# An expert window of one token tile gets a program of its own: tokens stationary, weights moving

## The reference

```python
# 1. decayed linear attention, per batch and head (4 x 8, 768 steps, width 64)
state = gamma * state + outer(k[t], v[t]);  y[t] = scale * q[t] @ state
# 2. mixture of 8 experts, the best one for each token (D = 512, F = 1024)
e_idx = argmax(x @ w_gate + modality_bias[modality_id])
for e in range(8):
    h = relu(x[e_idx == e] @ w1[e])
    out[e_idx == e] = gate * (h @ w2[e])
# 3. a bilinear block
out = (((x @ w1) * (x @ w2)) @ w3) @ w_out
```

## Time and profile before

| | before |
|---|---|
| median of 3 runs | 889.22 us (887.43 to 889.95) |
| the profiled execution | 886.92 us, its span 885.2 us |
| PE busy | 858.8 us, 97% of the span |
| ACT busy | 239.4 us, 27% |
| DVE busy | 288.0 us, 33% |
| granted PE clock, mean | 0.991 |
| instructions | 14799 |

### The profile page before, as it was taken

One profiled execution on the slowest core, in us unless ns is written; L12 is line 12 of the kernel. 1 busy time (PEld: TensorE's weight loads), 2 busy tenths in 40 slices (PEclk: granted clock), 3 DMA queues, 4 the chain that ended last, 5 costly groups with the idle time before them and its releaser, 6 DMA issues.

```text
span 885.2 us, 14799 instructions
## 1 busy us (share of the span) xinstructions
PE 858.8 (97%) x5854; PEld 741.6 (84%) x5855; DVE 288.0 (33%) x499; ACT 239.4 (27%) x388; POOL 89.0 (10%) x111
## 2 busy tenths in 40 slices
PE   9999999998989999999989999999999999999995
PEld 8899888788989998888878888888888888888884
DVE  3678698411121422121425430230230230220210
ACT  2234423311212432112334421221221231221210
POOL 3232003120202020202000001001001001001001
PEclk9999999999999999999999999999999999999998
DMA  9999871531112052303146002002002002001000
GB/s 342 339 333 305 310 261 50 186 97 52 49 48 71 30 184 95 95 0 95 40 149 191 1 1 95 1 1 95 0 1 94 0 10 85 0 0 48 1 12 36
DMA packets 43094, 84.16 MB, mean 95 GB/s; under 512 B 7345, under 2 KB 7473, under 8 KB 43057
## 3 DMA queue, kind: packets, MB, share of 16 engines
q1 hardware_dynamic: 33376, 60.08, 19.6%
q0 software_dynamic: 4736, 14.72, 5.2%
q10 hardware_dynamic: 4946, 8.86, 3.0%
HBM read 62.64 MB, written 21.00 MB: 94 GB/s over the span
## 4 chain that ended last, share of the span: by engine, by line
PE 93%; DVE 3%; issue 2%; ACT 0%; ACTq 0%; POOL 0%; DVEq 0%
PE bank L398 47%; PE attn L398 33%; PE bank L793 3%; PE attn L820 3%; PE pair L805 3%; PE pair L898 1%; PE bank L832 1%; PE attn L811 1%; PE bank L770 1%; PE bank L950 1%; DVE w3T L1020 0%; DVE we_p L1020 0%; PE pair L777 0%; ACTq L353 0%; DVE hT L1266 0%
## 5 line engine op out<-in xcount | busy, mean ns | idle before, releaser
L398 PE MATMUL bank<-yT,wab 128*128 128x512 f32 x1152 | 262.2, 389 | 1.7 <-issue 1.7
L398 PEld LDWEIGHTS bank<-yT,wab 128*128 128x128 f32 x1152 | 216.1, 188 | 46.7 <-issue 1.9
L398 PE MATMUL bank<-xT,we_p 128*128 128x512 f32 (+2 forms) x768 | 154.2, 361 | 11.7 <-issue 8.0
L398 PEld LDWEIGHTS bank<-xT,we_p 128*128 128x128 f32 x768 | 136.8, 192 | 28.7 <-issue 10.4
L398 PE MATMUL attn<-hT,we_p 128*128 128x512 f32 (+2 forms) x768 | 153.5, 357 | 0.0
L398 PEld LDWEIGHTS attn<-hT,we_p 128*128 128x128 f32 x768 | 132.9, 188 | 14.4
L398 PE MATMUL attn<-wc,gT 128*128 128x512 f32 x576 | 131.5, 389 | 0.0
L398 PEld LDWEIGHTS attn<-wc,gT 128*128 128x128 f32 x576 | 108.1, 188 | 22.5
L1305 DVE TENSOR_TENSOR g<-bank,acopy 128x512 f32<-128x512 f32 x48 | 33.2, 692 | 258.8 <-PE bank L398 258.8
L1266 DVE SCALAR_TENSOR_TENSOR hT<-bank,hT 128x512 fp32r<-128x512 f32 x64 | 44.1, 691 | 171.5 <-ACT hT L659 171.5
L659 ACT ACTIVATE hT<-bank 128x512 fp32r<-128x512 f32 x64 | 38.2, 598 | 114.1 <-PE bank L398 114.1
(11 more groups left out here) (156 smaller groups left out, 572.0 us busy)
## 6 DMA issues: line engine op xcount, KB each, us to landing
we_raw<-in_moe_w_dram SPq DMA_DIRECT2D x6, 2048.0 KB, 9.1
yT_sorted<-yout ACTq DMA_DIRECT2D x8, 1024.0 KB, 4.9
qkv<-in_q_t_dram SPq DMA_DIRECT2D x24, 256.0 KB, 3.7
qkv<-in_v_dram SPq DMA_DIRECT2D x24, 256.0 KB, 5.4
x_rows<-x_keep SPq DMA_DIRECT2D x24, 256.0 KB, 3.3
ytile<-yT_sorted SPq DMA_DIRECT2D x6, 1024.0 KB, 5.0
qkv<-in_k_t_dram SPq DMA_DIRECT2D x23, 256.0 KB, 5.3
qkv<-in_k_dram SPq DMA_DIRECT2D x20, 256.0 KB, 5.8
```

The lines of the kernel that those rows point to most:

```text
L398: i = pe.matmul(out_, left(a), right(b), start=(first and n == 0), stop=(last and n == 2), **kw)
```

## The change

The `wide(2)` program goes. A window of two tiles uses `wide(3)` (there is none with these inputs), and a window of one tile gets a program of its own, `one_tile`, on PE, and matching branches on ACT and DVE:

- PE: h is made as tokens by features: for each half of 512 features 12 matmuls with the 128 tokens of `xT` stationary and w1 moving, 512 columns, into bank 0 or 1. ACT copies the bank to `h_rows`, PE transposes its four 128 x 128 blocks back into the same bank, ACT takes relu (one instruction for four blocks) and DVE the low part. Then 24 matmuls with `hT` stationary and w2 moving, 512 columns, make y as tokens by features in bank 4. ACT copies it to `y_rows`, PE transposes four blocks into bank 5, ACT copies that to `yout`, and the store writes 128 columns instead of 512.
- ACT and DVE read `SIZE` at the head of every window and branch on it. In the one-tile branch `w2_hi`/`w2_lo` for pieces 0 and 1 stand ahead of the h copies, and pieces 2 and 3 behind relu.
- In every window, the load of "the next window begins a new expert" (`coming`) is moved from f = 5 to behind f = 7, and the load of the first row (`start`) from the last y copy to ahead of the first.

```diff
+        def columns_of(tensor, start, wide=BANK):
@@ act
-                for f in range(KF):
-                    h_hi(w, f)
-                    if f == 0:
-                        this = is_new(act, w)
-                    if f in (1, 3):
-                        if_new(act, this, w, lambda run: w2_hi(run, range(f - 1, f + 1)))
-                    if f == KF - 3:
-                        coming = is_new(act, w + 1)
+                def wide_hidden():
...
+                def one_tile_hidden():
+                    this = is_new(act, w)
+                    if_new(act, this, w, lambda run: w2_hi(run, range(0, 2)))
+                    for half in range(2):
+                        act.wait_ge(s_hp, w * KF + (half + 1))
+                        copy(h_rows[:, half * BANK:(half + 1) * BANK], bank[half][:, :]).then_inc(s_hhi, 1)
+                    for half in range(2):
+                        act.wait_ge(s_hp, w * KF + (half + 1) * (GT - 1) + 2)
+                        act.activation(hT[:, HI, half * GT:(half + 1) * GT, 0:P], bank[half][:, :].rearrange("p (f t) -> p f t", f=GT),
+                                       ACT.Relu).then_inc(s_hhi, GT - 1)
+                    if_new(act, this, w, lambda run: w2_hi(run, range(2, 4)))
+                def one_tile_outward():
+                    act.wait_ge(s_yp, w * KD + 1)
+                    copy(y_rows[:, :], bank[4][:, :]).then_inc(s_y, 2)
+                    with act.If(total > w + 1):
+                        x_hi(w + 1, range(KD))
+                    act.wait_ge(s_yst, w * 16 + 16)
+                    act.wait_ge(s_yp, w * KD + KD)
+                    copy(yout[:, :, 0:P], bank[5][:, :].rearrange("p (d t) -> p d t", d=KD)).then_inc(s_y, 2)
+                    y_store(w, start, P)
+                    with act.If(total < w + 2):
+                        wab_hi(2)
+                        wab_hi(3)
+                size = table(act, w, SIZE, 1, GT)
+                with act.If(size > 1):
+                    wide_hidden()
+                with act.If(size < 2):
+                    one_tile_hidden()
+                coming = is_new(act, w + 1)
                 if_new(act, coming, w + 1, w1_hi)
                 with act.If(total < w + 2):
                     for j in range(KD):
                         yT_hi(0, j)
                     wab_hi(0)
                     wab_hi(1)
+                start = start_row(act, w)
+                with act.If(size > 1):
+                    wide_outward()
+                with act.If(size < 2):
+                    one_tile_outward()
@@ pe
+                def one_tile():
+                    run = table(pe, w, RUN_OF, 0, E - 1)
+                    for half in range(2):
+                        pe.wait_ge(s_hlo, w * KF + (half + 1))
+                        for k in range(KD):
...
+                            i = product(pe, bank[half][:, :], lambda a: xT[:, a, k, 0:P], lambda a: we1_p[:, a, k, half * BANK:(half + 1) * BANK],
+                                        k == 0, k == KD - 1)
+                        i.then_inc(s_hp, 1)
+                    for half in range(2):
+                        pe.wait_ge(s_hhi, w * KF + (half + 1))
+                        for t in range(GT):
+                            i = pe.transpose(bank[half][:, t * P:(t + 1) * P], h_rows[:, half * BANK + t * P:half * BANK + (t + 1) * P], ident)
+                        i.then_inc(s_hp, GT - 1)
+                    pe.wait_ge(s_y, w * KD + 1)
+                    for f in range(KF):
+                        if f % GT == 0:
+                            pe.wait_ge(s_hlo, w * KF + (f + GT + 2))
+                        if f % 2 == 0:
+                            pe.wait_ge(s_w2lo, run * (KF // 2) + (f // 2 + 1))
+                        i = product(pe, bank[4][:, :], lambda a: hT[:, a, f, 0:P], lambda a: we2_p[:, a, f, :], f == 0, f == KF - 1)
+                    i.then_inc(s_yp, 1)
+                    with pe.If(total > w + 1):
+                        x_rows(w + 1, range(KD))
+                    pe.wait_ge(s_y, w * KD + 4)
+                    for d in range(KD):
+                        i = pe.transpose(bank[5][:, d * P:(d + 1) * P], y_rows[:, d * P:(d + 1) * P], ident)
+                    i.then_inc(s_yp, KD - 1)
                 size = table(pe, w, SIZE, 1, GT)
...
-                    with pe.If(size > 2):
+                    with pe.If(size > 1):
                         wide(3)
-                    with pe.If(size < 3):
-                        wide(2)
+                    with pe.If(size < 2):
+                        one_tile()
@@ dve
+                def one_tile_hidden():
+                    this = is_new(dve, w)
+                    if_new(dve, this, w, lambda run: w2_lo(run, range(0, 2)))
+                    for half in range(2):
+                        dve.wait_ge(s_hhi, w * KF + (half + 1) * (GT - 1) + 2)
+                        fs = slice(half * GT, (half + 1) * GT)
+                        dve.scalar_tensor_tensor(hT[:, LO, fs, 0:P], bank[half][:, :].rearrange("p (f t) -> p f t", f=GT), 0.0,
+                                                 hT[:, HI, fs, 0:P].bitcast(F32), ALU.max, ALU.subtract).then_inc(s_hlo, GT)
+                    if_new(dve, this, w, lambda run: w2_lo(run, range(2, 4)))
+                size = table(dve, w, SIZE, 1, GT)
```

More of the change, by code:

```diff
@@ L206, in build @@
         hT = r("hT", [P, 2, KF, BANK], F32R)
+        h_rows = r("h_rows", [P, FF])
+        y_rows = r("y_rows", [P, DM])
         wab = region(at_w)("wab", [P, 2, 2, 2 * KD, BANK], F32R)
@@ L368, in start_row @@
             return 0 if isinstance(w, int) and w == 0 else table(eng, w, START, 0, NT * P)
-        def columns_of(tensor, start):
-            cols = tensor[:, start:start + BANK] if isinstance(start, int) else tensor[:, bass.ds(start, BANK)]
+        def columns_of(tensor, start, wide=BANK):
+            cols = tensor[:, start:start + wide] if isinstance(start, int) else tensor[:, bass.ds(start, wide)]
             return cols.rearrange("(d p) c -> p d c", p=P)
@@ L665, in y_copy, with y_store @@
                 copy(yout[:, d, :], bank[4 + d % 2][:, :]).then_inc(s_y, 1)
-            def y_store(w, start):
+            def y_store(w, start, wide):
                 act.wait_ge(s_y, w * KD + (KD + 2))
-                act.dma_start(columns_of(yT_sorted, start), yout[:, :, :]).then_inc(s_yst, 16)
+                act.dma_start(columns_of(yT_sorted, start, wide), yout[:, :, 0:wide]).then_inc(s_yst, 16)
             def wab_hi(f):
@@ L682, in window @@
             def window(w, total):
-                for f in range(KF):
-                    h_hi(w, f)
-                    if f == 0:
-                        this = is_new(act, w)
-                    if f in (1, 3):
-                        if_new(act, this, w, lambda run: w2_hi(run, range(f - 1, f + 1)))
-                    if f == KF - 3:
-                        coming = is_new(act, w + 1)
+                def wide_hidden():
+                    for f in range(KF):
+                        h_hi(w, f)
+                        if f == 0:
+                            this = is_new(act, w)
+                        if f in (1, 3):
+                            if_new(act, this, w, lambda run: w2_hi(run, range(f - 1, f + 1)))
@@ new lines, in wide_outward @@
+                def wide_outward():
+                    for d in range(KD):
+                        y_copy(w, d)
+                        if d < KD // 2:
+                            with act.If(total > w + 1):
+                                x_hi(w + 1, range(2 * d, 2 * d + 2))
+                        if d == 0:
+                            with act.If(total < w + 2):
+                                wab_hi(2)
+                                wab_hi(3)
+                    y_store(w, start, BANK)
@@ L932, in wide @@
                                 x_rows(w + 1, range(2 * d, 2 * d + 2))
+                def one_tile():
[3 more added lines that the diff above has]
+                        for k in range(KD):
+                            if half == 0:
+                                pe.wait_ge(s_ixlo, w * KD + (k + 1))
+                                pe.wait_ge(s_w1lo, run * KD + (k + 1))
+                            i = product(pe, bank[half][:, :], lambda a: xT[:, a, k, 0:P], lambda a: we1_p[:, a, k, half * BANK:(half + 1) * BANK],
[7 more added lines that the diff above has]
+                    pe.wait_ge(s_y, w * KD + 1)
+                    for f in range(KF):
+                        if f % GT == 0:
[7 more added lines that the diff above has]
+                    pe.wait_ge(s_y, w * KD + 4)
+                    for d in range(KD):
+                        i = pe.transpose(bank[5][:, d * P:(d + 1) * P], y_rows[:, d * P:(d + 1) * P], ident)
+                    i.then_inc(s_yp, KD - 1)
                 size = table(pe, w, SIZE, 1, GT)
@@ L1283, in window, with wide_hidden @@
             def window(w, total):
```

(16 more changed lines are left out.)

## The result

| | before | after |
|---|---|---|
| median | 889.37 us (887.43 to 889.95, 4 runs) | 880.38 us (876.75 to 881.25, 4 runs) |
| ratio to before | | 0.9895, 95% interval 0.9863 to 0.9926 |
| the profiled execution, its span | 886.92, 885.2 us | 881.25, 879.5 us |
| from window 0's first matmul to the end | 728.4 us | 720.7 us |
| granted PE clock, mean | 0.991 | 0.987 |

The forecast was 882.5, and the change takes 9 us off. The two profiles differ by only 5.7 us, because window 0 began 2.0 us later in the one of after (158.83 and not 156.83). That part of the program was not changed, and its start wandered between 156.2 and 159.9 us over the profiles of this study. I therefore count from window 0's first matmul on: 885.2 - 156.8 = 728.4 and 879.5 - 158.8 = 720.7, **7.7 us** less.

The account below looks back on a forecast made before the run. PE, busy 858.8 of 885.2 us, was taken as the bound. Stage 3 starting 8.3 us earlier, less 1.6 for one clock drop, gave 6.7 off 889.2: 882.5 us, overall range 874.5 to 886.5.

Parts of the forecast that it names:

- rival A: Code fetch ahead of window 2: dropping skipped wide(2) removes the 5.12 us gap and its clock drop, 6.7 us; chance 0.27.
- the likeliest case: Gaps ahead of windows 1 and 2 stand, one clock drop: 882.5 us, range 880 to 884.5; chance 0.52.
- The signs of being wrong: Gaps at windows 1 and 2 change, window 7 to stage 3 outside 18 to 22 us, or wide-window relu over 0.3 late.
- Steps 1 to 3: Window 7's h products, ACT's loads and copies, transposes, relu: PE waits 2.2 us for ACT; y products start at 465.45.
- Step 4: Window 7's y products: from 465.45 to 471.2, w2 pieces 2 and 3 just in time, margin under 0.3 us.
- the earlier pair of waits: PE's waits of 2.2 and 0.9 us in window 7, 461.1 to 465.45: second clock-drop candidate, left out of the sum.
- Step 5: End of window 7: ACT copies y behind stage-3 work and loads, so PE waits 1.9 us.
- Step 6: Loop end ahead of stage 3: 1.72 us of issue stays, at worst 5.12; stage 3 starts 8.3 us earlier.
- Step 7: Waits of 3.6 in 4.3 us right ahead of stage 3 bring one drop of PE's clock, costing 1.6 us.
- The wide windows: Seven windows of 384 or 512 columns: added and moved register loads cost 0, bound 2 us; dropping wide(2) costs nothing.
- Rival B: Window 7: second clock drop (1.6 us), exit 3.4 longer, or late w2 piece or load; 885.8 us; chance 0.15.
- Rival C: ACT's and DVE's longer loops fetch code in seven windows: 7 to 25 us, less 6.7; 896.5 us; chance 0.06.

Follow-up runs that it names:

- e5: Changed kernel with all four w2 pieces of the one-tile window moved behind relu and the low part, on ACT and DVE; 879.39 us, ratio 0.9910.
- e6: Changed kernel with ACT's and DVE's branch taken from the number of windows, without loading SIZE for it; 876.58 us, ratio 0.9883.
- e3: Changed kernel with matmuls of unused result put into PE's four waits of the one-tile window; 874.17 us, ratio 0.9863.
- e1: Changed kernel with the 256-column program put back in PE's loop body, where nothing runs it; 884.23 us, ratio 0.9976.
- e4: Changed kernel with all engines' window loops run exactly eight turns, without the five empty ones; 871.18 us, ratio 0.9808.
- e8: Kernel before with the window loops run exactly eight turns, without the five empty ones; 884.13 us, ratio 0.9964.
- e0: Kernel before, unchanged, run again for a second profile; 887.19 us.
- e2: Kernel before with only the 256-column program taken out, so the one-tile window runs the 384-column one; 886.72 us, ratio 0.9997.
- e10: Changed kernel, unchanged, run again for a second profile; 878.99 us, ratio 0.9891.
- e9: Changed kernel with exactly eight loop turns and filling matmuls in only PE's first three one-tile-window waits; 870.03 us, ratio 0.9803.
- e7: Changed kernel with both exactly eight loop turns and filling matmuls in PE's four one-tile-window waits; 870.62 us, ratio 0.9802.

## Why the prediction was right, point by point

The time, the sign and the range were right. The way there was right in part, and that the sum came within 2.1 us is luck, since two misses cancelled: the sum had 8.3 - 1.6 = 6.7 us from window 7 and the clock, which gave 5.4 - 2.9 = 2.5; rival A, which I had left out of the likeliest case, gave 6.3. The signs of being wrong that the prediction named did come. The gap at window 2 changed, and window 7 to stage 3 took 22.99 us, outside 18 to 22.

1. **Steps 1 to 3, the h half**: right. ACT's pieces began 3.8 us behind the store's issue (3.9 in the sum), PE waited 2.07 (2.2), and the y products began 9.9 us after the window's start (10.0). The remark that the order of ACT's branch costs most there was wrong: e5 turned it round and won nothing. The single price of a load, 1.0 us, was right for the first and too high for the next ones: taking one away gave 0.5 in e6.
2. **Step 4, the y products**: 8.36 us in place of 5.7. The term was missing because I left the earlier pair of waits out of the clock's account. In e3 and e1, where the clock stayed up, they took 5.78, so the products themselves and the just-in-time pieces of w2 were costed rightly.
3. **Step 5, the wait for the y copy**: 0.75 and not 1.9, and not only because the y products ended late: in e1 and e6, where they took 5.78 and 5.74, it was 0.75 too. ACT's loads of `coming` and `start` cost nothing, since its four `yT_hi` followed the w2 pieces at once (463.96, the pieces from 462.05, 2.00 long): those loads run beside its instructions. In the profile of after ACT even waited 2.51 us for PE.
4. **Step 6, the way out**: 3.35 and not 1.72, the failed step with the largest consequence. I had named both ends and taken the wrong one. The measured 1.72 was, by the simplest reading, what remained of the loop's end behind queued matmuls, and the new window ends with four short transposes. e4 and e8 show it from both sides: the same edit removes 3.35 in one kernel and 1.72 in the other.
5. **Step 7, the clock**: mechanism right, size wrong. Two spells and not one, and longer: 4 and 5 us had a mean of 0.69 and 0.66 in the earlier trace rows, and 5 and 6 us stayed at 0.50 in after. They cost 2.7 and 2.9 us, not 1.6 once. e3 removed both.
6. **The wide windows**: taken at 0, bound 2 us; the `SIZE` load showed 0.2 to 0.4 us in windows 2 and 3, gone in e6. `wide(2)`, "costs nothing when dropped", was the wrong sentence in the sum: its place in PE's loop body had cost 6.3 us, as rival A said.
7. **Rival A** (0.27) happened, by the mechanism given and at nearly the price given (6.7). **Rival B** (0.15), the second spell and the longer way out, happened too. I had treated them as cases that exclude each other, while they lie in different windows: the right list had a fourth entry, both at once, at the prices given 882.5 - 6.7 + 1.6 + 1.7 = 879.1, close to the 880.4 measured. **Rival C** (0.06) didn't happen: from window 3 to window 6 of after the longest "issue" wait of ACT is 1.0 us, ahead of the w1 pieces, where the load of `coming` now stands, and DVE has none. PE's longest wait there is 0.4 us.

The Trainium skill's rule behind C (Runtime: NRT & Kernel Launch, Instruction fetch mechanics), that a taken branch to code outside the pages held forces a fetch, agrees in kind with e0, e1 and e2: a program that is only skipped makes a gap of 4.3 to 5.1 us on PE, and the code queue moves more there. As to every turn it doesn't: between the windows from 3 to 7, with the same kind of turns and skips, no kernel here has an "issue" gap of even half a us.

## What to carry to other kernels

Before costing a branch that nobody takes at nothing, look at the "issue" gaps of the engine that is the bound: here the code that was skipped was worth more (6.3 us) than the code that was changed (2.5), and a loop run for its exact number of turns as much again in the changed kernel (3.35 and, through the clock, 3.1), though only 3.1 us in the kernel before. A gap measured behind a long row of queued matmuls is only what they left uncovered; where the new program ends in a few short instructions, take the whole. And when two rivals lie in different places, add a case in which both happen.

## What the runs showed of the hardware that I had not expected

- The empty turns of a loop on PE: 5 turns and the exit cost 3.4 us behind four transposes and 1.7 behind 96 matmuls of 256 columns, and nothing when they were left out.
- The lower clock comes in spells of differing length from the same waits: the y products took 8.38, 7.33, 8.21 and 8.15 us in after, e10, e4 and e5, and 5.78 and 5.74 in e1 and e6, with waits of about 2 and 1 us ahead of them in after, e10 and e1, 2.06 and 0.69 in e4, 1.54 and 1.07 in e6, 0.25 and 3.35 in e5. The waits of after and of e1 agree within 0.1 us and the y products don't.
- Ahead of window 1, gaps of 2.06, 2.29 and 2.45 us (e9, e8, e5) left its 96 matmuls at 16.91 to 16.93 us, and gaps of 2.74 to 3.53 us (e4, e7, e2, before, e1, e3, e0, e10, e6, after) were followed by 18.2 to 19.7. So a few tenths more in a gap went with 1.3 us and more behind it. That may be part of why the runs of one kernel scatter by 4 us; no run here shows it.
